# Regrouping the retention stage of a fused retention, MLP and gated-attention kernel into steps of whole head pairs

## The chip, the cores and the metric

One core of a Trainium2 chip runs the whole program. The metric is the device time of one execution in microseconds (us). The core has five engines that run side by side, each in its own order: TensorE (PE, matrix products; its weight loads are shown apart as PEld), VectorE (DVE), ScalarE (ACT), GpSimd (POOL), and SyncE (SP), which here only issues DMA transfers. Engines wait for each other on semaphores. Matrix products land in PSUM, eight banks of 512 fp32 columns in each of 128 partitions; DVE and ACT read PSUM, everything else lies in SBUF.

## The reference, cut to what matters

Three blocks follow one another. The change touches only the first, a retention (linear attention with decay) over 2 batches, 8 heads, 768 positions and 64 channels a head:

```python
gamma = 1.0 - 2.0 ** (-5.0 - np.arange(H))
for t in range(S):
    state = gamma * state + einsum('bhd,bhe->bhde', k[:, :, t], v[:, :, t])
    y[:, :, t] = scale * einsum('bhd,bhde->bhe', q[:, :, t], state)
x = y.transpose(0, 2, 1, 3).reshape(B, S, H * D)
# then: x + relu(layernorm(x) @ w_ch1) @ w_ch2, and a top-2 gated mixture of four causal attentions
```

All of it is fp32. The second block (layer norm, hidden layer of 2048, back to 512) starts when the retention's output is there.

## The kernel before

The retention is done in chunks of 128 positions (six a sequence). The decay is folded into the rows of q and k beforehand (`scale_rows`, L295: `scaled_k`, `scaled_q`), so inside a chunk the result is a causally masked score matrix times v, and over chunks it is q times a running sum of the chunks' k-v products. Two heads (a pair) lie side by side in the 128 partitions, so there are eight pairs (`NIT` = 8), and the six chunks of a pair are worked in two groups of three (`g` = 0, 1). For every pair `it`, TensorE does

- `turn(it, unit)`, L616: transposes of `scaled_k` and `scaled_q`, four units of three 128x128 tiles (units 0 and 1 belong to group 0, 2 and 3 to group 1). ACT copies each unit out of PSUM (`turned`, L956, into `k_t` and `q_t`).
- `scores_of(it, g)`, L629: three chunks x two heads, each a product over 64 rows (the array shape that the profile writes 64*128), the two heads side by side. DVE multiplies them by the causal mask (`apply_causal`, L1175, into `prob`).
- `chunk_outputs(it, g)`, L642: `prob` times v, each head into 64 of the 128 columns (shape 128*64), side by side.
- `key_values(it)`, L674: outer products k-v of five chunks x two heads, also 128*64. DVE makes the running sums from them (`states`, L1184 and L1187).
- `state_outputs(it, g)`, L649: q times the running sum, on the full array (128*128), added onto the chunk outputs in PSUM. ACT copies the sum out to `x` (`y_out`, L962).

An fp32 product appears in the profile as two matmul records and a transpose as one: 12 records for the scores or the chunk outputs of a group, 20 for `key_values`, 4 and 6 for the state outputs of groups 0 and 1, 3 for a transpose unit.

The order is written out by hand on every engine. Before the change the groups of two neighbouring pairs are interleaved: scores (it, 1), chunk outputs (it, 0), state outputs (it, 0), transposes of the next pair, scores (it+1, 0), chunk outputs (it, 1), key-values (it+1), state outputs (it, 1), transposes. Transposes use PSUM banks 0 and 1 in turn, all scores banks 2 and 3, outputs banks 4 and 5, key-values banks 6 and 7.

The rows of q, k and v come by DMA from SP (`load_heads`, L409), three pairs deep; `raw_v` of pair n is loaded once the state outputs of pair n-3 are finished (`s_y`). GpSimd scales the rows of pairs 2 to 7 (L295), then splits the weights of the MLP into high and low parts (L497 to L507); the splits of the second weight matrix start when all of `x` is out (`s_yx`). A first mean over channels (`first_mean`, L657), `first_centre` (L1244), `first_hi` (L974) and `first_lo` (L1250) prepare the MLP's first input tiles, and `hidden(0, 0)` (L723) is the MLP's first product. From there TensorE runs the MLP without a pause.

Of the kernel before, what the change touches and what calls it, by code (L numbers as in the profile page):

```python
# [70 lines left out]
def retention_moe_program(nc, q, k, v, g_ln, w_ch1, w_ch2, w_gate, wq, wk, wv, wo, out):  # L71
# [30 lines left out]
    with ExitStack() as ctx:  # L102
# [55 lines left out]
        with ExitStack() as r:  # L158
            raw = {n: sb(r, f"raw_{n}", [P, RB, 2, NC, D]) for n in "qkv"}
            scaled = {n: sb(r, f"scaled_{n}", [P, RB, NC, 2 * D]) for n in "qk"}  # L160
            k_t = sb(r, "k_t", [P, 2, NC, P])
            q_t = sb(r, "q_t", [P, 2, NC, P])
            prob = sb(r, "prob", [P, 2, 2, G, P])
            state = sb(r, "state", [P, 2, NC - 1, P])

        with ExitStack() as m:
            w2 = {part: sb(m, f"w2_{part}", [P, NF, DM], F32R) for part in ("hi", "lo")}
            h_t = {part: sb(m, f"h_t_{part}", [P, 2, N], F32R) for part in ("hi", "lo")}
            xn_t = {part: sb(m, f"xn_t_{part}", [P, KT, N], F32R) for part in ("hi", "lo")}
            rows = sb(m, "rows", [P, B, KT, U, P])  # L170
# [433 lines left out]
        def _(pe):  # L604

            def turn(n, unit):

                which, g = T_UNITS[unit]
                pe.wait_ge(s_scaled[which], 2 * n + g + 1)
                if unit >= 2:  # L610

                    pe.wait_ge(s_turned, 4 * n + unit - 1)
                elif n >= 1:
                    pe.wait_ge(s_turned, 4 * (n - 1) + unit + 3)
                for c in range(G):
                    mm = pe.transpose(t_bank(unit)[:, c * P:(c + 1) * P], scaled[which][:, n % RB, G * g + c, :],  # L616
                                      ident[:, :])
                mm.then_inc(s_t, 1)

            def scores_of(it, g):  # L620

                pe.wait_ge(s_turned, 4 * it + 2 * g + 2)
                if 2 * it + g >= 1:

                    pe.wait_ge(s_prob, 2 * it + g)
                for c in range(G):
                    for j in range(2):
                        rows = slice(j * D, (j + 1) * D)
                        mm = pe.matmul(s_bank()[:, j, c], k_t[rows, it % 2, G * g + c, :],  # L629
                                       q_t[rows, it % 2, G * g + c, :], start=True, stop=True)  # L630
                mm.then_inc(s_s, 1)

            def chunk_outputs(it, g):

                wait_loaded(pe, it, "v", g)
                pe.wait_ge(s_prob, 2 * it + g + 1)
                if it >= 1:
                    pe.wait_ge(s_yx, y_turn(it - 1, g) + 1)
                for c in range(G):
                    for j in range(2):  # L640
                        rows_ = slice(j * D, (j + 1) * D)
                        pe.matmul(y_bank(g)[rows_, c * P:(c + 1) * P], raw["v"][:, it % RB, j, G * g + c], prob[:, g, j, c, :],  # L642
                                  start=(c == 0), stop=(g == 0 and c == 0), skip_group_check=True)

            def state_outputs(it, g):

                pe.wait_ge(s_st, (NC - 1) * (it + 1))
                for c in range(max(1, G * g), G * g + G):
                    mm = pe.matmul(y_bank(g)[:, (c - G * g) * P:(c - G * g + 1) * P], state[:, it % 2, c - 1, :],  # L649
# [3 lines left out]
            def first_mean(b):  # L653

                pe.wait_ge(s_const, 5)
                pe.wait_ge(s_acc, (HP - 1) * (b + 1))
# [29 lines left out]
            for it in range(NIT - 1):  # L686

                scores_of(it, 1)
                chunk_outputs(it, 0)
                if it == NIT - 2:  # L690
                    key_values(it + 1)
                state_outputs(it, 0)
                if it == HP + 1:
                    first_mean(0)
                for unit in range(0 if it == 0 else 2, 4):
                    turn(it + 1, unit)

                scores_of(it + 1, 0)
                chunk_outputs(it, 1)
                if it < NIT - 2:  # L700
                    key_values(it + 1)
                    state_outputs(it, 1)
                    for unit in (0, 1):
                        turn(it + 2, unit)

            chunk_outputs(NIT - 1, 0)
            state_outputs(NIT - 1, 0)
            state_outputs(NIT - 2, 1)
            scores_of(NIT - 1, 1)
            first_mean(1)  # L710
            chunk_outputs(NIT - 1, 1)
            state_outputs(NIT - 1, 1)
# [45 lines left out]
            hidden(0, 0)  # L758
            hidden(0, 1)
            pe.wait_ge(s_yx, 2 * NIT)  # L760
# [186 lines left out]
        def _(act):  # L947
# [11 lines left out]
            def y_out(it, g):  # L959

                act.wait_ge(s_y, y_turn(it, g) + 1)
                act.activation(x[:, it, G * g:G * g + G, :].rearrange("p c t -> p (c t)"), y_bank(g),  # L962
# [21 lines left out]
            for it in range(NIT - 2):  # L984
                y_out(it, 0)
                for unit in range(0 if it == 0 else 2, 4):
                    turned(it + 1, unit)
                y_out(it, 1)
                for unit in (0, 1):
                    turned(it + 2, unit)  # L990
                if it == HP + 1:
                    for kk in range(KT):
                        first_hi(0, kk)
            y_out(NIT - 2, 0)
            for unit in (2, 3):
                turned(NIT - 1, unit)
            y_out(NIT - 1, 0)
            y_out(NIT - 2, 1)
            for kk in range(KT):
                first_hi(1, kk)  # L1000
            y_out(NIT - 1, 1)
# [166 lines left out]
        def _(dve):  # L1168

            def apply_causal(it, g):  # L1170
                dve.wait_ge(s_s, 2 * it + g + 1)
                if it >= 1:

                    dve.wait_ge(s_y, y_turn(it - 1, g) + 1)
                dve.tensor_tensor(prob[:, g], s_bank(),  # L1175
# [22 lines left out]
            states(0)  # L1198

# [144 lines left out]
            for it in range(NIT - 1):  # L1344
                apply_causal(it, 1)
                if it == 0:
                    dve.wait_ge(s_tab_rest, 16)
                    for g in range(2):
                        for n in "kq":
                            scale_rows(dve, 1, n, g)  # L1350
                if it == NIT - 2:
                    states(it + 1)
                b, kk = divmod(it - 1, HP)
                if it >= 2 and kk > 0:
                    first_sum(b, kk)
                if it == HP + 1:
                    for kk in range(KT):
                        first_centre(0, kk)
                apply_causal(it + 1, 0)
                if it < NIT - 2:  # L1360
                    states(it + 1)
            first_sum(1, HP - 2)
            for kk in range(KT):
                first_lo(0, kk)
            first_sum(1, HP - 1)
            apply_causal(NIT - 1, 1)
# [192 lines left out]
```

## Time and profile before

| | |
|---|---|
| median of 3 runs | 471.7 us (471.1 to 472.78) |
| the profiled execution | 470.56 us, of which the span is 468.8 us |
| PE busy | 456.1 us (97%) |
| DVE, ACT, POOL busy | 269.7, 149.9, 153.2 us |
| retention: first transpose to first MLP product | 5.1 to 64.3 us of the span |
| granted TensorE clock | 1.00 throughout |

The span goes from the first to the last instruction; the rest of the time of the execution lies around it. A busy PE is one that always has a matmul in flight. A matmul's record lasts longer than it blocks the next, so a group's duration in the timeline overlaps the following group; the chain of waits, in which each piece ends where the next begins, shows what a group really takes.

### The profile page before, as it was taken

Reading aid. Unit: us, or ns where it says so; the run is one execution under the profiler, and the core shown is the slowest. Engines: PE = TensorE matmul, PEld = TensorE weight load, DVE = VectorE, ACT = ScalarE, POOL = GpSimd, SP = SyncE. Lnnn points to the kernel's source line nnn. Section 1 sums busy time; section 2 is a strip of 40 time slices with the busy share of each in tenths; the row PEclk is TensorE's granted clock in tenths of the full one; section 3 lists DMA queues with packets and bytes.
Section 4 is the critical chain, followed back from the end, with each engine's and each line's share of the span. In section 5 each row is a group of like instructions: output and inputs, shape, how many; then the busy total and the mean of one; then the engine's idle time right before and its main releaser. Section 6 shows DMA issues by size and latency. Waiting matters only on the chain.

```text
span 468.8 us, 7454 instructions
## 1 busy us (share of the span) xinstructions
PE 456.1 (97%) x2762; PEld 392.8 (84%) x2762; DVE 269.7 (58%) x599; ACT 149.9 (32%) x343; POOL 153.2 (33%) x190
## 2 busy tenths in 40 slices
PE   7999999999999999999999999999999899999896
PEld 6788878888888888888888888888999799998775
DVE  4555761186515388732265785144438889888833
ACT  2434431111113111111131111132435777777823
POOL 1474438998900000000002000000501667666710
PEclk9999999999999999999999999999999999999999
DMA  7997504344200000000040000000155444442024
GB/s 170 245 216 161 142 23 136 112 136 134 67 1 1 0 0 0 0 0 0 0 101 13 0 1 0 0 2 0 24 127 123 119 117 107 99 103 68 1 111 159
DMA packets 65792, 33.04 MB, mean 70 GB/s; under 512 B 47584, under 2 KB 61920, under 8 KB 65760
## 3 DMA queue, kind: packets, MB, share of 16 engines
q1 hardware_dynamic: 64960, 32.43, 26.8%
q8 instruction: 19, 0.31, 0.3%
q10 hardware_dynamic: 800, 0.20, 0.2%
q14 instruction: 13, 0.11, 0.1%
HBM read 20.03 MB, written 3.15 MB: 49 GB/s over the span
## 4 chain that ended last, share of the span: by engine, by line
PE 87%; DVE 5%; ACT 2%; issue 2%; SPq 1%; DMA 1%; POOL 1%; POOLq 0%; ACTq 0%; DVEq 0%
PE ps L723 28%; PE ps L732 28%; PE ps L807 5%; PE ps L858 4%; PE ps L779 3%; PE ps L826 3%; PE ps L642 3%; PE ps L629 3%; PE ps L841 2%; PE ps L649 2%; PE ps L885 2%; PE ps L616 2%; DVE a L1439 2%; SPq L445 1%; DVE a_low_lo L1447 1%
## 5 line engine op out<-in xcount | busy, mean ns | idle before, releaser
L1290 DVE SCALAR_TENSOR_TENSOR h_t_lo<-ps,h_t_hi 128x512 fp32r<-128x512 f32 x48 | 33.2, 692 | 124.5 <-ACT h_t_hi L1011 124.5
L1011 ACT ACTIVATE h_t_hi<-ps 128x512 fp32r<-128x512 f32 x48 | 28.7, 598 | 216.7 <-PE ps L723 216.7
L723 PE MATMUL ps<-xn_t_hi,w_hi 128*128 128x512 f32 x192 | 74.9, 390 | 0.0
L723 PE MATMUL ps<-xn_t_lo,w_hi 128*128 128x512 f32 x192 | 74.8, 390 | 0.0
L732 PE MATMUL ps<-w_hi,h_t_lo 128*128 128x512 f32 x192 | 74.8, 390 | 0.0
L723 PE MATMUL ps<-xn_t_hi,w_lo 128*128 128x512 f32 x192 | 74.8, 390 | 0.0
L732 PE MATMUL ps<-w_hi,h_t_hi 128*128 128x512 f32 x192 | 74.8, 390 | 0.0
L732 PE MATMUL ps<-w_lo,h_t_hi 128*128 128x512 f32 x192 | 74.8, 390 | 0.0
L574 POOL TENSOR_SCALAR a<-a,inv_den,weight 128x768 f32<-128x768 f32 (+5 forms) x48 | 34.0, 717 | 50.6 <-DVE inv_den L1459 50.3
L723 PEld LDWEIGHTS ps<-xn_t_hi,w_hi 128*128 128x128 f32 x192 | 36.1, 188 | 7.6
L723 PEld LDWEIGHTS ps<-xn_t_hi,w_lo 128*128 128x128 f32 x192 | 36.1, 188 | 7.5
L732 PEld LDWEIGHTS ps<-w_hi,h_t_lo 128*128 128x128 f32 x192 | 36.1, 188 | 7.5
L732 PEld LDWEIGHTS ps<-w_hi,h_t_hi 128*128 128x128 f32 x192 | 36.1, 188 | 7.5
L732 PEld LDWEIGHTS ps<-w_lo,h_t_hi 128*128 128x128 f32 x192 | 36.1, 188 | 7.4
L723 PEld LDWEIGHTS ps<-xn_t_lo,w_hi 128*128 128x128 f32 x192 | 36.1, 188 | 7.3
L537 POOL TENSOR_SCALAR w_vg_hi<-raw_vg 128x1040 fp32r<-128x1040 f32 x1 | 1.1, 1061 | 118.5 <-DMA raw_wo<-in_moe_wo 118.5
L1066 ACT ACTIVATE a<-a,neg_max 128x768 f32<-128x768 f32 (+5 forms) x48 | 32.3, 674 | 13.9 <-DVE neg_max L1439 13.9
L1277 DVE STREAM_TRANSPOSE rows<-x 32x512 f32<-32x512 f32 x48 | 33.7, 702 | 1.4
L1439 DVE CUSTOM_DVE_ANT_0 a<-ps,masked 128x768 f32<-128x768 f32 (+5 forms) x48 | 27.8, 616 | 0.3 <-PE ps L826 0.3
L841 PE MATMUL ps<-ident,a 128*128 128x128 f32 x168 | 23.6, 277 | 3.5 <-DVE a_low_lo L1447 2.4
L545 POOL TENSOR_SCALAR raw_qk<-raw_qk 128x256 f32<-128x256 f32 x4 | 1.6, 405 | 77.4 <-PE ps L732 76.7
L841 PEld LDWEIGHTS ps<-ident,a 128*128 128x128 f32 x168 | 18.6, 141 | 6.6 <-POOL a L574 5.0
(146 smaller groups left out, 891.2 us busy)
## 6 DMA issues: line engine op xcount, KB each, us to landing
raw_w<-in_moe_w_ch SPq DMA_DIRECT2D x32, 256.0 KB, 2.9
k_twice_hi<-pj_hi SPq DMA_DIRECT2D x32, 96.0 KB, 2.2
k_twice_lo<-pj_lo SPq DMA_DIRECT2D x32, 96.0 KB, 2.2
out_y<-out_sb SPq DMA_DIRECT2D x12, 256.0 KB, 2.0
raw_k<-in_k SPq DMA_DIRECT2D x7, 384.0 KB, 4.7
raw_q<-in_q SPq DMA_DIRECT2D x7, 384.0 KB, 5.2
raw_v<-in_v SPq DMA_DIRECT2D x7, 384.0 KB, 3.8
q_both<-pj_hi SPq DMA_DIRECT2D x16, 96.0 KB, 2.1
```

What stands on the lines that cost most here:

```text
L574: pool.tensor_scalar(a[:, g % AB, c0:c1], a[:, g % AB, c0:c1], inv_den[:, u:u + 1], weight[:, u, e:e + 1], ALU.mult, ALU.mult).then_inc(s_ ...
L629: mm = pe.matmul(s_bank()[:, j, c], k_t[rows, it % 2, G * g + c, :], q_t[rows, it % 2, G * g + c, :], start=True, stop=True)
L723: mm = pe.matmul(ps[:, f % 2, :], w1[a_][:, f, kk, :], xn_t[b_][:, kk, :], start=(kk == 0 and p_ == 0), stop=(kk == KT - 1 and p_ == 2))
L732: mm = pe.matmul(ps[:, 2 + tau, :], h_t[a_][:, f % 2, tau * P:(tau + 1) * P], w2[b_][:, f, :], start=(f == 0 and p_ == 0), stop=(f == NF - ...
L807: mm = pe.matmul(pj_bank(n), w_qk[a_][n // 4 % 2][:, kk, :], x2[b_][:, b, kk, half_cols(n)], start=(kk == 0 and p_ == 0), stop=(kk == KT - ...
L841: mm = pe.transpose(flat(4, 6, s0 + P)[:, s0:s0 + P], a[:, g % AB, s0:s0 + P], ident[:, :])
L858: mm = pe.matmul(z_bank(top)[:, skip:HALF], ev[:, b * NC + sc, e].rearrange("p h d -> p (h d)"), (a_top if top else a_low)[part][:, sc, sk ...
L1011: act.activation(h_t["hi"][:, f % 2, :], ps[:, f % 2, :], ACT.Relu).then_inc(s_hhi, 1)
L1066: act.activation(a[:, g % AB, c0:c1], a[:, g % AB, c0:c1], ACT.Exp, bias=neg_max[:, 2 * (g % AB) + w:2 * (g % AB) + w + 1], scale=-1.0, ac ...
L1277: dve.transpose(rows[quad(a_), :, :, :, quad(d_)].rearrange("p b k u d -> p (b k) u d"), x[quad(d_), :, U * n:U * n + U, quad(a_)]).then_i ...
L1290: dve.scalar_tensor_tensor(h_t["lo"][:, f % 2, :], ps[:, f % 2, :], 0.0, f32(h_t["hi"][:, f % 2, :]), ALU.max, ALU.subtract).then_inc(s_hl ...
L1439: dve.tensor_tensor_reduce(a[:, g % AB, c0:c1], sc_bank(g, c1)[:, c0:c1], masked[:, NC - 1 - i:NC, :].rearrange("p c t -> p (c t)"), -1.0, ...
```

## The change

The retention runs in steps of a whole pair. A step's order on TensorE is: scores of both groups of pair `it`, chunk outputs of both groups of the pair before, key-values of `it`, state outputs of both groups of the pair before, the four transpose units of pair `it+1`. Pair 0 is finished before step 1 begins, and pairs 6 and 7 are finished together at the end. Transpose units take banks 0 to 3, one each, and the scores of group g banks 2g and 2g+1; so a transpose now waits for the masking (`s_prob`) that reads the scores in its banks, and `prob` is kept for two pairs. ACT and DVE follow: ACT copies out both output groups and then the four units, DVE masks both groups and then makes the running sums. The outputs of pair 7 go to banks 0 and 1, so the wait for all of `x` moves ahead of `hidden(0, 1)`. `rows` and `xn_t` change places in SBUF.

```diff
-            prob = sb(r, "prob", [P, 2, 2, G, P])
+            prob = sb(r, "prob", [P, 2, 2, 2, G, P])
...
         def t_bank(unit):
-            return ps[:, unit % 2, 0:G * P]
+            return ps[:, unit, 0:G * P]
-        def s_bank():
-            return ps[:, 2:4, 0:G * P].rearrange("p j (c t) -> p j c t", c=G)
+        def s_bank(g):
+            return ps[:, 2 * g:2 * g + 2, 0:G * P].rearrange("p j (c t) -> p j c t", c=G)
-        def y_bank(g):
-            return ps[:, 4 + g, 0:G * P]
+        def y_bank(it, g):
+            return ps[:, (0 if it == NIT - 1 else 4) + g, 0:G * P]
...
                 pe.wait_ge(s_scaled[which], 2 * n + g + 1)
-                if unit >= 2:
-                    pe.wait_ge(s_turned, 4 * n + unit - 1)
-                elif n >= 1:
-                    pe.wait_ge(s_turned, 4 * (n - 1) + unit + 3)
+                if n >= 1:
+                    pe.wait_ge(s_prob, 2 * n - 1 + unit // 2)
...
                 pe.wait_ge(s_turned, 4 * it + 2 * g + 2)
-                if 2 * it + g >= 1:
-                    pe.wait_ge(s_prob, 2 * it + g)
...
             key_values(0)
-            for it in range(NIT - 1):
-                scores_of(it, 1)
-                chunk_outputs(it, 0)
-                if it == NIT - 2:
-                    key_values(it + 1)
-                state_outputs(it, 0)
+            scores_of(0, 1)
+            for g in range(2):
+                chunk_outputs(0, g)
+                state_outputs(0, g)
+            for unit in range(4):
+                turn(1, unit)
+            for it in range(1, NIT - 1):
+                for g in range(2):
+                    scores_of(it, g)
+                if it > 1:
+                    for g in range(2):
+                        chunk_outputs(it - 1, g)
+                key_values(it)
+                if it > 1:
+                    for g in range(2):
+                        state_outputs(it - 1, g)
+                for unit in range(4):
+                    turn(it + 1, unit)
                 if it == HP + 1:
                     first_mean(0)
-                for unit in range(0 if it == 0 else 2, 4):
-                    turn(it + 1, unit)
-                scores_of(it + 1, 0)
+            for g in range(2):
+                scores_of(NIT - 1, g)
+            key_values(NIT - 1)
+            for it in (NIT - 2, NIT - 1):
+                chunk_outputs(it, 0)
+            for it in (NIT - 2, NIT - 1):
+                state_outputs(it, 0)
+            for it in (NIT - 2, NIT - 1):
                 chunk_outputs(it, 1)
...
             first_mean(1)
-            chunk_outputs(NIT - 1, 1)
-            state_outputs(NIT - 1, 1)
+            for it in (NIT - 2, NIT - 1):
+                state_outputs(it, 1)
...
             hidden(0, 0)
+            pe.wait_ge(s_yx, 2 * NIT)
             hidden(0, 1)
-            pe.wait_ge(s_yx, 2 * NIT)
...
-            for it in range(NIT - 2):
-                y_out(it, 0)
-                for unit in range(0 if it == 0 else 2, 4):
-                    turned(it + 1, unit)
-                y_out(it, 1)
-                for unit in (0, 1):
-                    turned(it + 2, unit)
+            for it in range(1, NIT):
...
+                if it != 2:
+                    for g in range(2):
+                        y_out(max(0, it - 2), g)
+                for unit in range(4):
+                    turned(it, unit)
...
-            for it in range(NIT - 1):
-                apply_causal(it, 1)
...
-                apply_causal(it + 1, 0)
-                if it < NIT - 2:
-                    states(it + 1)
+            for it in range(1, NIT):
...
+                apply_causal(it, 0)
+                if it < NIT - 1:
+                    apply_causal(it, 1)
+                states(it)
...
+            apply_causal(NIT - 1, 1)
             first_sum(1, HP - 2)
-            for kk in range(KT):
-                first_lo(0, kk)
             first_sum(1, HP - 1)
-            apply_causal(NIT - 1, 1)
```

On TensorE, the order of one whole period in the middle of the retention before (one group of pair `it`, then the other; the name says what is read, `q_t,k_t` are scores, `prob,raw_v` chunk outputs, `raw_v,scaled_k` key-values, `q_t,state` state outputs, `ident,...` transposes):

```order
L629 MATMUL ps<-q_t,k_t 128x128 x6
L642 MATMUL ps<-prob,raw_v 64x128 x6
L649 MATMUL ps<-q_t,state 128x128 x2
L616 MATMUL ps<-ident,scaled_k 128x128 x3
L616 MATMUL ps<-ident,scaled_q 128x128 x3
L629 MATMUL ps<-q_t,k_t 128x128 x6
L642 MATMUL ps<-prob,raw_v 64x128 x6
L674 MATMUL ps<-raw_v,scaled_k 64x64 x10
L649 MATMUL ps<-q_t,state 128x128 x3
L616 MATMUL ps<-ident,scaled_k 128x128 x3
L616 MATMUL ps<-ident,scaled_q 128x128 x3
```

and the same place after:

```order
L623 MATMUL ps<-q_t,k_t 128x128 x12
L636 MATMUL ps<-prob,raw_v 64x128 x12
L670 MATMUL ps<-raw_v,scaled_k 64x64 x10
L643 MATMUL ps<-q_t,state 128x128 x5
L613 MATMUL ps<-ident,scaled_k 128x128 x3
L613 MATMUL ps<-ident,scaled_q 128x128 x3
L613 MATMUL ps<-ident,scaled_k 128x128 x3
L613 MATMUL ps<-ident,scaled_q 128x128 x3
```

The same instructions stand there, but scores, chunk outputs and state outputs come once in a period instead of twice, and all transposes of a pair stand directly ahead of its scores.

On ACT in the same place, before (`k_t` and `q_t` are the transposes' copies, `x` an output group's):

```order
L962 ACTIVATE x<-ps 128x384
L956 ACTIVATE k_t<-ps 128x384
L956 ACTIVATE q_t<-ps 128x384
L962 ACTIVATE x<-ps 128x384
L956 ACTIVATE k_t<-ps 128x384
L956 ACTIVATE q_t<-ps 128x384
```

and after:

```order
L965 ACTIVATE x<-ps 128x384 x2
L959 ACTIVATE k_t<-ps 128x384
L959 ACTIVATE q_t<-ps 128x384
L959 ACTIVATE k_t<-ps 128x384
L959 ACTIVATE q_t<-ps 128x384
```

Six copies stand in a row now, the outputs' ahead of the four of the transposes.

## Rows read from the trace of the kernel before

**Rows 1.** The page, busy time, share of the span and instructions of each engine
```profile
PE 456.1 (97%) x2762; PEld 392.8 (84%) x2762; DVE 269.7 (58%) x599; ACT 149.9 (32%) x343; POOL 153.2 (33%) x190
```
**Rows 2.** Chain of waits, 24 to 31 us: start, us until the next piece, what
```profile
24.22 0.87 PE ps L649 x6
25.08 0.65 PE ps L616 x6
25.74 0.87 PE ps L629 x12
26.61 0.81 PE ps L642 x12
27.41 0.64 PE ps L649 x4
...
30.38 0.58 PE ps L674 x20
```
**Rows 3.** Windows, one period: us, busy PE PEld DVE ACT POOL, clock, DMA
```profile
24.90:31.70 6.80, 6.80 (x93) 5.99 (x92) 3.74 (x9) 2.51 (x6) 4.51 (x6) 1.00 1.01 231
```
**Rows 4.** Timeline of PE: start, us, line, out<-in, array shape, count
```profile
24.15 0.94 PE L649 MATMUL ps<-q_t,state 128*128 128x128 f32 x6
...
26.54 0.88 PE L642 MATMUL ps<-prob,raw_v 128*64 128x128 f32 x12
...
27.34 0.71 PE L649 MATMUL ps<-q_t,state 128*128 128x128 f32 x4
...
29.51 0.88 PE L642 MATMUL ps<-prob,raw_v 128*64 128x128 f32 x12
...
30.21 0.75 PE L674 MATMUL ps<-raw_v,scaled_k 128*64 128x64 f32 x20
```
**Rows 5.** Timeline of ACT's copies out of PSUM, and one handoff to PE
```profile
6.12 0.49 ACT L956 ACTIVATE q_t<-ps 128x384 f32<-128x384 f32 x1
...
6.66 0.94 PE L629 MATMUL ps<-q_t,k_t 64*128 64x128 f32 x12 [0.58 <-ACT q_t L956]
...
25.12 0.49 ACT L962 ACTIVATE x<-ps 128x384 f32<-128x384 f32 x1 [2.52 <-PE ps L649]
...
25.51 0.48 ACT L956 ACTIVATE k_t<-ps 128x384 f32<-128x384 f32 x1
...
25.88 0.50 ACT L956 ACTIVATE q_t<-ps 128x384 f32<-128x384 f32 x1
```
**Rows 6.** Timeline of DVE, running sums and masking
```profile
24.59 1.27 DVE L1187 TENSOR_TENSOR state<-ps,state 128x128 f32<-128x128 f32 x4
...
26.65 0.96 DVE L1175 TENSOR_TENSOR prob<-ps,causal 128x768 f32<-128x768 f32 x1 [0.80 <-PE ps L629]
```
**Rows 7.** Timeline of the start, 11 to 20 us
```profile
11.36 0.95 DVE L1175 TENSOR_TENSOR prob<-ps,causal 128x768 f32<-128x768 f32 x1
...
13.76 0.55 DVE L295 TENSOR_TENSOR scaled_q<-raw_q,decay_sb 128x384 f32<-128x384 f32 x1
...
19.14 0.83 POOL L295 TENSOR_TENSOR scaled_q<-raw_q,decay_sb 128x384 f32<-128x384 f32 x1
```
**Rows 8.** Timeline of SP and POOL, one load and the scaling behind it
```profile
38.61 0.37 SPq L409 DMA_DIRECT2D raw_v<-in_v  x1
...
47.71 0.83 POOL L295 TENSOR_TENSOR scaled_q<-raw_q,decay_sb 128x384 f32<-128x384 f32 x1
```
**Rows 9.** Timeline of the end of the retention
```profile
61.67 0.70 PE L657 MATMUL ps<-head_sum,mean_of 128*128 128x256 f32 x2
...
62.66 0.74 DVE L1244 TENSOR_TENSOR centred<-x,ps 128x256 f32<-128x256 f32 x2
...
62.84 0.88 PE L642 MATMUL ps<-prob,raw_v 128*64 128x128 f32 x12 [0.48 <-issue]
...
64.34 0.47 PE L723 MATMUL ps<-xn_t_hi,w_hi 128*128 128x512 f32 x1
...
66.20 0.62 POOL L505 TENSOR_SCALAR w_hi<-raw_w 128x512 fp32r<-128x512 f32 x1 [12.09 <-ACT x L962]
```

More of the change, by code:

```diff
@@ L168, in retention_moe_program @@
             h_t = {part: sb(m, f"h_t_{part}", [P, 2, N], F32R) for part in ("hi", "lo")}
+            rows = sb(m, "rows", [P, B, KT, U, P])
             xn_t = {part: sb(m, f"xn_t_{part}", [P, KT, N], F32R) for part in ("hi", "lo")}
-            rows = sb(m, "rows", [P, B, KT, U, P])
             stats = sb(m, "stats", [P, NT, 2, 6])
@@ L628, in scores_of @@
                         rows = slice(j * D, (j + 1) * D)
-                        mm = pe.matmul(s_bank()[:, j, c], k_t[rows, it % 2, G * g + c, :],
+                        mm = pe.matmul(s_bank(g)[:, j, c], k_t[rows, it % 2, G * g + c, :],
                                        q_t[rows, it % 2, G * g + c, :], start=True, stop=True)
@@ L648, in state_outputs @@
                 for c in range(max(1, G * g), G * g + G):
[L649 removed]
+                    mm = pe.matmul(y_bank(it, g)[:, (c - G * g) * P:(c - G * g + 1) * P], state[:, it % 2, c - 1, :],
                                    q_t[:, it % 2, c, :], start=False, stop=True, skip_group_check=True)
@@ L983, in _ @@
                 turned(0, unit)
-            for it in range(NIT - 2):
-                y_out(it, 0)
-                for unit in range(0 if it == 0 else 2, 4):
-                    turned(it + 1, unit)
-                y_out(it, 1)
-                for unit in (0, 1):
-                    turned(it + 2, unit)
-                if it == HP + 1:
+            for it in range(1, NIT):
+                if it == HP + 3:
                     for kk in range(KT):
                         first_hi(0, kk)
[L994 to L998, printed above, removed]
+                if it != 2:
[3 more added lines that the diff above has]
+                    turned(it, unit)
+            for it in (NIT - 2, NIT - 1):
+                y_out(it, 0)
             for kk in range(KT):
                 first_hi(1, kk)
-            y_out(NIT - 1, 1)
+            for it in (NIT - 2, NIT - 1):
+                y_out(it, 1)
             def xn_hi(n, kk):
@@ L1198, in _ @@
             states(0)
+            apply_causal(0, 1)
+            dve.wait_ge(s_tab_rest, 16)
+            for g in range(2):
+                for n in "kq":
+                    scale_rows(dve, 1, n, g)
             def normalise(n):
@@ L1342, in mlp @@
                     hidden_lo(i + 1, 1)
-            for it in range(NIT - 1):
-                apply_causal(it, 1)
[L1346 to L1351, printed above, removed]
-                    states(it + 1)
-                b, kk = divmod(it - 1, HP)
+            for it in range(1, NIT):
+                if it == HP + 2:
+                    for kk in range(KT):
+                        first_centre(0, kk)
+                if it == HP + 3:
+                    for kk in (2, 3):
+                        first_lo(0, kk)
+                b, kk = divmod(it - 2, HP)
                 if it >= 2 and kk > 0:
                     first_sum(b, kk)
-                if it == HP + 1:
-                    for kk in range(KT):
-                        first_centre(0, kk)
-                apply_causal(it + 1, 0)
-                if it < NIT - 2:
-                    states(it + 1)
+                apply_causal(it, 0)
+                if it < NIT - 1:
+                    apply_causal(it, 1)
+                states(it)
+                if it == HP + 2:
+                    for kk in (0, 1):
+                        first_lo(0, kk)
+            apply_causal(NIT - 1, 1)
             first_sum(1, HP - 2)
-            for kk in range(KT):
-                first_lo(0, kk)
             first_sum(1, HP - 1)
-            apply_causal(NIT - 1, 1)
             first_centre(1, 0)
```

21 lines of the change are left out of this document (8 added, 13 removed).

## The prediction, made before the changed kernel was run

> **What bounds the kernel now.** I read the page's busy shares first, then the chain of waits through the retention, then PE's timeline in it. The page has PE busy for 97% of the span [rows 1], so only what shortens PE's own work or its pauses can shorten the kernel. The chain of waits runs through nothing but PE in the middle of the retention, and in one period there (two groups of a pair) PE is busy for the whole stretch, ACT for 2.5 us of 6.8 [rows 3]. The reader should see in [rows 2] that pieces of like work cost unlike times. State outputs take 0.64 us for four records and 0.87 for six, so a record costs 0.11 and 0.20 to 0.21 is left over. Six transposes take 0.65, which is 6 x 0.11 with nothing over. Twelve score records, two side by side, are six slots of 0.11 and take 0.87: 0.21 over. Chunk outputs are also six slots and take 0.81: 0.15 over. The key-values take 0.58 for ten slots of half width, nothing over. What the three with something over share is that each begins with another array shape than the work ahead of it had: full array to 64*128, to 128*64, back to the full array. The two without follow work of their own shape. [Rows 4] shows it with the same work twice: chunk outputs go on to key-values, of their own shape, after 0.70 us (29.51 to 30.21), but to state outputs, of another, after 0.80 (26.54 to 27.34); the rest of the extra sits behind the first record of the new shape. So a change of shape costs about 0.10 as a pause and 0.05 to 0.10 in the first product.
>
> The sum of a period: 2 x 0.87 + 2 x 0.81 + 0.58 + 0.64 + 0.87 + 2 x 0.65 = 6.75, of which 2 x (0.21 + 0.15 + 0.20) = 1.1 us is changes of shape.
>
> The Trainium skill, page "TensorEngine Tiling (Array Packing)", section Tiling Modes, says that a change of the tiling mode, unlike a change of tile, drains the engine. By that rule grouping by shape saves whatever the drains cost, and the rows above give the price; the same page's section Performance Considerations speaks against the change, see the first rival.
>
> **The steady step.** The change keeps every instruction and halves the changes of shape: 6.75 - 0.55 = 6.2 us a step if PE still never waits. Laid out from the first score at 0: scores to 1.44, pause, chunk outputs 1.54 to 2.91, key-values to 3.49, pause, state outputs 3.59 to 4.81, transposes to 6.12, next scores at 6.22.
>
> Does anything make PE wait?
> - Masking (DVE): group 0's scores are done at about 0.93, group 1's at 1.61; each masking takes 0.96 [rows 6], so both are done by 2.9. The transposes that now wait for it, and behind which everything on PE would queue, come at 4.81. Hidden.
> - Running sums (DVE): key-values are done at 3.66, the sums take 0.3 + 1.27 [rows 6] and end at 5.3; the state outputs that need them come in the next step at 3.6. Hidden.
> - Copies (ACT): this is the tight one. Before, the transposes of a group stood about 3 us ahead of the scores that use them; now the scores of group 0 come directly behind. The last state output is done at 4.97 (a record is in flight for 0.28: 24.15 + 0.94 less the start of the last record, 5 x 0.11 + 0.1 behind the first) [rows 4]. Both output copies stand ahead of the transposes' on ACT. ACT starts a copy 0.03 after the product is done (24.15 + 0.94 against 25.12) [rows 4, 5] and a next one 0.39 and 0.37 after the last, although each is shown as 0.48 to 0.50 [rows 5]. So: second output copy at 5.01, first k copy at 5.40, first q copy at 5.77, done at 6.26, and PE starts 0.05 later as at 6.12 + 0.49 = 6.61 against 6.66 [rows 5]: 6.31. The scores start at 6.31 instead of 6.22: 0.1 us a step is given back. Group 1's copies are done at 7.0, its scores are due at 7.08: hidden.
>
> So a step takes 6.3 us. The upper bound of this unknown: if six copies in a row went one after the other at 0.49, group 0's would be done at 6.48 and group 1's at 7.46; the scores of group 0 would start at 6.53, those of group 1 at 7.5 instead of 7.3, and a step would cost 6.75. The lower bound is 6.2. I take 6.3, since a pitch of 0.37 to 0.39 is what three copies in a row show, the third of which was ready to go before ACT was.
>
> **Start.** Nothing changes up to the masking of pair 0's second group. The second chunk outputs of pair 0 wait for the masking of 11.36 + 0.95 = 12.31 [rows 7]: 12.36 to 13.07; state outputs 13.17 to 13.94. The transposes of pair 1 follow at 13.94; their rows are all scaled by 13.76 + 0.55 = 14.31, the last unit's 0.6 us ahead of its turn, so PE no longer waits unit by unit. They end at 15.25; the copies behind the two output copies free the scores at 15.44. Scores to 16.89, key-values to 17.6. The transposes of pair 2 then wait for GpSimd's scaling, which is bound by its loads and does not move: its last unit is scaled at 19.14 + 0.83 = 19.97 [rows 7], so they end at 20.35 and step 2 starts at 20.44. Bounds: 20.3 and 20.9 (a load or the copies later).
>
> **Steps 2 to 6.** 20.44 + 6.31 = 26.75, then 33.06 and 39.37. Step 5 has the first mean (two records of 256 columns, 0.44 at 0.11 for 128) behind the transposes, which also gives ACT time to catch up: 39.37 + 6.22 + 0.43 = 46.02. Its centring (four operations on DVE, two of which take 0.74 [rows 9], so 1.4) makes the maskings of step 6 0.8 us later, against 2.4 us of slack. Step 7 starts at 52.33.
>
> **End.** Steps of the last order, from 52.33: scores to 1.44, key-values 1.54 to 2.17, chunk outputs of group 0 of both pairs to 3.49, state outputs 3.59 to 4.59 (the sums of pair 7 are done at 4.0, hidden), chunk outputs of group 1 4.69 to 6.05 (masking done at 4.9, hidden, where the kernel before waits at 62.84 [rows 9]), mean 6.15 to 6.69, state outputs to 8.03. The centring can start 0.05 behind the mean's 0.70 in flight [rows 9], at 6.90; before, the MLP's first product came 64.34 - 62.66 = 1.68 behind the first centring [rows 9], with PE as the last to be ready; without that I count 1.55: 8.45. PE waits 0.4 us there for the first input tile. The first product is at 52.33 + 8.45 = 60.8 instead of 64.34: 3.5 us earlier.
>
> **Behind it.** The wait for all of `x` ahead of `hidden(0, 1)`: the split that waits for it started 66.20 - 62.66 = 3.54 behind the first centring [rows 9]; with one more copy (0.39) it is 3.93, less 1.55 is 2.4 us behind the first product, whose group of twelve needs 2.7: hidden by 0.3. GpSimd's split itself takes 0.62 and a second part of about twice that, to 4.3; it is needed at 5.5: hidden. The loads' order on SP is unchanged; `raw_v` of pair n is released a step later by its order, but steps are shorter. From the MLP on PE is the bound as before, so the 3.5 us reach the end. The swap in SBUF costs nothing, since no transfer or operand changes in size. In the profiled execution: span 468.8 - 3.5 = 465.3, time 470.56 - 3.5 = 467.1. That execution lies 1.1 us under the median of the runs, so from the median 471.7 - 3.5 = **468.2 us**.
>
> **Rivals.**
> - *The copies pace the step* (15%). The upper bound above: 0.45 us more in each of steps 2 to 4 and 6, and 0.3 at the start and the end: 2.1 us given back, 470.3 us or a little less. For it: a copy is shown as 0.49, and six in a row are nowhere in the trace. Against it: the pitch of three. Even so it is not slower than before. The page "TensorEngine Tiling (Array Packing)" of the Trainium skill, section Performance Considerations, warns that tiling speeds up the products but not the copies out of PSUM, which may become the bound; here the trace has ACT busy for 2.5 of 6.8 us [rows 3], so by load they do not; the bound above is one of latency, at one place.
> - *The extra belongs to the start of a group, not to the shape* (7%). Each group also starts with a wait on a semaphore. Then a step stays at 6.75 and only the start and the end gain: 471.3 us. Against it: the transposes behind state outputs and the key-values behind chunk outputs start with such waits too and have nothing over.
> - *The loads fall behind* (5%), the one on the slower side. A pair's v load now waits for outputs that finish one step later in the order, and k and q of the next pair queue behind it on SP, GpSimd's scaling behind them, and the transposes behind that. Before, the scaling for pair 7 ends 47.71 + 0.83 - 38.61 = 9.9 us after that v load was issued [rows 8]. After, the v load goes out 5.0 into a step and the last transposes that need the scaling are due 5.8 into the step two later: 2 x 6.3 + 0.8 = 13.4 us. It decides once that chain takes over 13.4; with 15.5 us for each of the pairs 5 to 7 it costs over 6 us and ends at 474 us. Against it: 3.5 us of slack.
> - *Less is lost than I count* (8%): the steps run at 6.2 and the end's wait of 0.4 is filled: 0.4 + 0.4 more, 467.4 us.
>
> **Numbers.** My forecast, with small errors of either sign, has 65%; its own range is 467.2 to 469.3. With the first rival inside, the range is 466.8 to 470.8. About 0.3% (1.4 us) is what a measurement of this kernel can tell from none. Faster by more (under 470.3): the forecast, the last rival and two thirds of the first: 0.84. Within: 0.11. Slower: 0.05.
>
> **What would show it.** In PE's timeline: one group of 24 score records, 24 of chunk outputs, 20, 10 and 12 in a row, at a distance of 6.2 to 6.4 us from step to step, the pieces 1.5, 1.4, 0.6, 1.2 and 1.3. A pause named after ACT's `q_t` of about 0.1 (wrong if 0.3 or more) ahead of the scores, the first score of step 2 near 20.4, the first MLP product near 60.8. Steps of 6.7 without waits would refute the price of the shapes; waits for `scaled_k` or `scaled_q` behind step 2 would show the loads.

## The result, and the profile after

The changed kernel is slower by 0.5%: 474.38 us (median of 8 runs, 472.57 to 476.1) against 472.19 us of the kernel before beside it (8 runs, 471.1 to 473.26), a ratio of 1.0047 [1.0026, 1.0069]. The prediction was 468.2 us, faster. The profiled execution took 474.35 us with a span of 472.6.

The page's line of busy time, which answers to [rows 1], gives PE half a microsecond less work in a span 3.8 us longer. So PE waits more, or the marks at both ends moved:

```profile
PE 455.6 (96%) x2762; PEld 394.4 (83%) x2762; DVE 268.8 (57%) x599; ACT 149.6 (32%) x343; POOL 153.6 (32%) x190
```

I then read the chain of waits of the changed kernel. Its middle, which answers to [rows 2]:

```profile
27.62 1.71 PE ps L623 x24
29.33 1.46 PE ps L636 x24
30.79 0.58 PE ps L670 x20
31.37 1.31 PE ps L643 x10
32.68 1.31 PE ps L613 x12
...
34.02 1.71 PE ps L623 x24
...
48.28 5.25 DMA g_col<-in_moe_g_ln
...
53.96 1.29 ACT xn_t_hi L977 x3
55.26 0.75 ACT x L965 x2
56.00 0.38 ACT k_t L959
56.38 0.39 ACT q_t L959
...
56.81 2.41 PE ps L623 x24
59.22 1.26 PE ps L670 x20
```

The reader is to see two things. In the middle a step is 6.40 us (27.62 to 34.02), against 6.75 before, and its pieces are close to the ones that were forecast. At 45.5 us the chain leaves PE, which it never did there before. It goes through SP's issues to the load of `g_col`, the gain of the layer norm (512 numbers), from there to `first_hi` on ACT, the two output copies, two transposes' copies, and only then to PE's scores of pair 7. Those 24 score records take 2.41 us instead of 1.71, and the 20 key-values 1.26 instead of 0.58.

One step by windows of the changed kernel, which answers to [rows 3] (us, busy PE, PEld, DVE, ACT, POOL, clock, DMA). ACT is as busy as before, 2.51 us, now in 6.40:

```profile
27.60:34.00 6.40, 6.37 (x90) 5.92 (x90) 3.86 (x8) 2.51 (x7) 4.75 (x6) 1.00 0.81 185
```

The timeline of the changed kernel, which answers to [rows 4 to 9]: the start and the end of step 2, the wait, and the first MLP product:

```profile
19.95 0.83 POOL L295 TENSOR_TENSOR scaled_q<-raw_q,decay_sb 128x384 f32<-128x384 f32 x1
...
21.32 1.61 PE L623 MATMUL ps<-q_t,k_t 64*128 64x128 f32 x24
...
26.31 0.49 ACT L965 ACTIVATE x<-ps 128x384 f32<-128x384 f32 x1 [0.18 <-PE ps L643]
26.70 0.49 ACT L959 ACTIVATE k_t<-ps 128x384 f32<-128x384 f32 x1
27.07 0.50 ACT L959 ACTIVATE q_t<-ps 128x384 f32<-128x384 f32 x1
27.44 0.51 ACT L959 ACTIVATE k_t<-ps 128x384 f32<-128x384 f32 x1
27.62 1.71 PE L623 MATMUL ps<-q_t,k_t 64*128 64x128 f32 x24
27.81 0.53 ACT L959 ACTIVATE q_t<-ps 128x384 f32<-128x384 f32 x1
...
47.02 0.53 ACT L959 ACTIVATE q_t<-ps 128x384 f32<-128x384 f32 x1
...
53.55 1.71 ACT L977 ACTIVATE xn_t_hi<-centred,g_col 128x256 fp32r<-128x256 f32 x4 [6.00 <-DMA g_col<-in_moe_g_ln]
...
56.81 2.41 PE L623 MATMUL ps<-q_t,k_t 64*128 64x128 f32 x24 [3.38 <-ACT q_t L959]
...
66.96 0.47 PE L726 MATMUL ps<-xn_t_hi,w_hi 128*128 128x512 f32 x1 [0.33 <-DVE xn_t_lo L1255]
```

ACT is done with pair 6's transposes at 47.5, reaches `first_hi` and stands there for 6.00 us until `g_col` is in. Behind it in ACT's order are the output copies of pair 5 and all transposes' copies of pair 7, so PE stands for 3.38 us. In the kernel before, `first_hi` stood behind the output copies of pair 5 and the first two transposes' copies of pair 7. The same load was issued at about the same time there (48.13 against 48.28) and landed after 4.2 us, at 52.3; ACT came to `first_hi` at 53.66 and found it there (timeline of before, no time in brackets ahead of the last row):

```profile
48.13 0.43 SPq L452 DMA_DIRECT2D g_col<-in_moe_g_ln  x1
...
53.66 1.71 ACT L974 ACTIVATE xn_t_hi<-centred,g_col 128x256 fp32r<-128x256 f32 x4
```

Windows of 2 us of the changed kernel, PE alone (us, busy PE, granted clock, DMA share, GB/s):

```profile
54.00:56.00 2.00, 0.00 (x0) 1.00 0.45 130
56.00:58.00 2.00, 1.19 (x16) 0.90 0.00 0
58.00:60.00 2.00, 2.00 (x28) 0.50 0.00 0
60.00:62.00 2.00, 2.00 (x34) 0.75 0.00 0
```

After the pause the granted clock stays full for the first records, falls to 0.50 (1.2 of 2.4 GHz) for somewhat over 3 us and comes back at 61. That is why the score and key-value records of step 7 take longer. The Trainium skill, page "TensorE: Matmul & The Clock Gate", section What's actually happening, says that TensorE is throttled to half its clock unless it has lately been active; the trace agrees, the fall comes behind a pause of 3.38 us (`e2` below has one behind shorter waits).

The first MLP product comes at 66.96 instead of 64.34 [rows 9], 2.6 us later, and every later piece of PE is shifted by the same 2.6. The other 1.2 us by which the two spans differ lie behind the last work of DVE (468.24 + 0.69 us against 465.60 + 0.69), in the last output transfer, which the order doesn't touch.

### The profile page after: what moved, and what is told of

It is laid out like the page before. It is cut to its first block, busy times and chain, and to the rows that moved or that the text cites. A ratio compares the mean times of both kernels' runs of the same rounds, so it can differ in the third digit from the quotient of the medians.

```text
span 472.6 us, 7436 instructions
## 1 busy us (share of the span) xinstructions
PE 455.6 (96%) x2762; PEld 394.4 (83%) x2762; DVE 268.8 (57%) x599; ACT 149.6 (32%) x343; POOL 153.6 (32%) x190
## 4 chain that ended last, share of the span: by engine, by line
PE 82%; DVE 5%; SPq 3%; DMA 3%; ACT 3%; issue 2%; POOL 1%; POOLq 0%; ACTq 0%; DVEq 0%
PE ps L726 28%; PE ps L735 28%; PE ps L810 5%; PE ps L861 4%; PE ps L782 3%; PE ps L829 3%; PE ps L844 2%; PE ps L888 2%; PE ps L623 2%; PE ps L636 2%; DVE a L1441 2%; PE ps L643 1%; DMA raw_q<-in_q 1%; DMA g_col<-in_moe_g_ln 1%; SPq L445 1%
## 5 line engine op out<-in xcount | busy, mean ns | idle before, releaser
L1066 ACT ACTIVATE a<-a,neg_max 128x768 f32<-128x768 f32 (+5 forms) x48 | 32.3, 674 | 13.9 <-DVE neg_max L1441 13.9
```

What stands on the lines that cost most here:

```text
L1066: act.activation(a[:, g % AB, c0:c1], a[:, g % AB, c0:c1], ACT.Exp, bias=neg_max[:, 2 * (g % AB) + w:2 * (g % AB) + w + 1], scale=-1.0, ac ...
```

## The experiments

Each has a short name, in brackets in its heading. The ratio of each is to the kernel before on the same chip (471.59 us, 35 runs, and 471.68, 29 runs, for `e4`, `e6`, `e8` and `e9`). The marks "..." in the diffs stand for lines left out. Times inside a kernel are from its profile; two marks serve throughout, the first score of step 7 and the first MLP product, 56.81 and 66.96 in the changed kernel.

**The load of `g_col` earlier, in the changed kernel (`e1`).** The load goes behind those of pair 5.

```diff
                 load_heads(it)
+                if it == 5:
...
+                        sp.dma_start(g_col[:, :], g_ln.rearrange("(k p) -> p k", p=P)).then_inc(s_gcol, 16)
...
-                sp.dma_start(g_col[:, :], g_ln.rearrange("(k p) -> p k", p=P)).then_inc(s_gcol, 16)
```

> The changed kernel with one edit: the 2 KB load of the gains g_col is issued behind the loads of pair 5 instead of behind the loads of the weights. Theory (the wait for g_col): in the changed kernel ACT's first_hi(0, 0) stands ahead of the output copies of pair 5 and the four transposes' copies of pair 7, and waited for g_col until 53.5 us; PE then had nothing to do for 3.4 us and came back at the lower clock. Expected: no wait for g_col, no pause ahead of step 7, granted clock 1.00 throughout, first MLP product at about 47.2 + 6.4 + 8.5 = 62.1 us instead of 66.96, so 4.9 us less than the changed kernel: about 469.5 us, 0.6% under the kernel before. Rival (the new order itself starves PE, the load is only what came last): the pause stays or moves, 473 to 474.5 us.

Measured: 469.82 us, ratio 0.9964 [0.9951, 0.9978]. One small transfer turns 0.5% slower into 0.4% faster. Step 7 starts at 53.36, 3.45 us earlier, and the first MLP product stands at 62.80, 4.16 earlier; the clock is full throughout. From the timeline of this kernel:

```profile
47.67 1.71 ACT L978 ACTIVATE xn_t_hi<-centred,g_col 128x256 fp32r<-128x256 f32 x4 [0.24 <-DVE centred L1250]
...
52.26 3.32 DVE L1256 SCALAR_TENSOR_TENSOR xn_t_lo<-centred,g_col,xn_t_hi 128x256 fp32r<-128x256 f32 x4
...
56.92 0.88 PE L637 MATMUL ps<-prob,raw_v 128*64 128x128 f32 x12 [0.47 <-DVE prob L1176]
...
62.80 0.47 PE L727 MATMUL ps<-xn_t_hi,w_hi 128*128 128x512 f32 x1 [0.33 <-DVE xn_t_lo L1256]
```

`first_hi` waits 0.24 us instead of 6.00. But the end, from 53.36, takes 9.44 us, not the 8.45 forecast: the four `first_lo` on DVE take 3.32 us, and behind them the masking of pair 7 is late, for which PE waits 0.47. This is the subject of `e8`.

**The load as it is, its users later, in the changed kernel (`e2`).** ACT's and DVE's work on the first batch's input tiles goes behind the loop over the pairs.

```diff
             for it in range(1, NIT):
-                if it == HP + 3:
-                    for kk in range(KT):
-                        first_hi(0, kk)
...
+            for kk in range(KT):
+                first_hi(0, kk)
             for it in (NIT - 2, NIT - 1):
                 y_out(it, 0)
...
-                        first_lo(0, kk)
...
             first_sum(1, HP - 1)
+            for kk in range(KT):
+                first_lo(0, kk)
```

> The changed kernel with g_col loaded where it was, but its users moved: first_hi(0, .) on ACT behind all transposes' copies, first_lo(0, .) on DVE behind the last first_sum. Theory (the wait for g_col): g_col still lands at about 53.5 us, but nothing that PE needs stands behind it on ACT, so step 7 starts at about 53.6 with the clock at 1.00; the four first_lo at the end make the last centring 0.4 to 0.5 us later: first MLP product at about 62.5, 469.9 us. Rival (the new order starves PE by itself): 473 to 474.5 us.

Measured: 470.13 us, ratio 0.9968 [0.9954, 0.9982]. Step 6 takes 6.31 us (49.14 to 55.45) instead of 9.65, at full clock. The load isn't harmful in itself; what stands behind its user in ACT's order is. The first MLP product is at 64.47, 1.67 later than in `e1`, and the reason lies at the start, as the timeline and a window of this kernel show:

```profile
21.89 2.94 PE L623 MATMUL ps<-q_t,k_t 64*128 64x128 f32 x24
...
22.00:24.00 2.00, 2.00 (x20) 0.50 1.15 262
```

The second step begins 0.68 us later than in `e1` (21.89 against 21.21) and takes 7.71 us instead of 6.30, since the granted clock is 0.50 for some 3.4 us of it. Ahead of it PE had waited three times for GpSimd's scaled rows, 1.00, 0.24 and 0.24 us; `e9` has waits of 0.54, 0.75, 0.24 and 0.24 us there and keeps its clock at 1.00. The end is 0.42 shorter than in `e1` (9.02 against 9.44), although PE waits 0.76 for the last input tiles. This execution (471.65 us) and one of 471.8 us have a mean granted clock of 0.995, the other ten of 0.997 or more, and they took 470.92 us or less. So most of them are without that fall.

**The same earlier load in the kernel before (`e3`).** The diff is that of `e1`.

> The kernel before with g_col issued behind the loads of pair 5. Theory (the wait for g_col): there g_col had landed at 52.3 us and its first user came at 53.66, so the wait was covered by 1.3 us and taking it earlier is worth nothing: the same 472.2 us within 0.3%. Rival (the small load disturbs the large ones around it, wherever it is put): a difference of 0.5 us or more either way, and loads of pair 6 that land later.

Measured: 471.57 us, ratio 1.0002 [0.999, 1.0014]. So an earlier `g_col` is worth nothing in the old order, and all that it gives in `e1` belongs to the new one.

**The load later in the kernel before (`e4`).** Its issue waits until the running sums of pair 6 are there.

```diff
+            sp.wait_ge(s_st, (NC - 1) * (HP + 3))
                 sp.dma_start(g_col[:, :], ...)
```

> The kernel before with g_col issued only when the running sums of pair 6 are done (about 53.3 us) instead of at 48.1. Theory (an early user on ACT exposes a late load, in either order): it lands at about 56, first_hi(0, 0) waits from 53.7 to 56, the output copy and the transposes' copies behind it on ACT come some 2 us later than at 56.1, and PE waits for them: 1.5 to 3 us slower than the kernel before, 473 to 474.6. Rival (the order before has so much slack behind first_hi that a late load costs nothing, the new order alone is to blame): within 0.3% of the kernel before.

Measured: 471.1 us, ratio 0.9997 [0.998, 1.0015]. The timeline of this kernel:

```profile
53.12 0.37 SPq L453 DMA_DIRECT2D g_col<-in_moe_g_ln  x1
...
55.23 1.71 ACT L975 ACTIVATE xn_t_hi<-centred,g_col 128x256 fp32r<-128x256 f32 x4 [1.63 <-DMA g_col<-in_moe_g_ln]
56.85 0.47 ACT L963 ACTIVATE x<-ps 128x384 f32<-128x384 f32 x1
```

ACT does wait for `g_col`, 1.63 us, and it costs nothing: the output copy behind it starts at 56.85 instead of 56.09, and the first MLP product is at 64.16. I had held that the load is exposed in either order once it is late; that fell as far as this run goes. In the old order ACT has idle time behind `first_hi`, and PE wants the transposes' copies late: the last of them is done at 58.07, and the scores that read it start at 60.61. The delay came out shorter than meant, since the lone load landed in 2.1 us; a longer one was not tried.

**The pause filled, in the changed kernel (`e5`).** PE makes 30 transposes into a free part of a bank while it waits. The wait for `g_col` stays.

```diff
                     first_mean(0)
+            pe.wait_ge(s_st, (NC - 1) * (NIT - 1))
+            pe.wait_ge(s_xc, KT)
+            for _ in range(30):
+                pe.transpose(ps[:, 7, 3 * P:4 * P], ident[:, :], ident[:, :])
             for g in range(2):
                 scores_of(NIT - 1, g)
```

> The changed kernel with 30 transposes of the identity into a free part of bank 7 ahead of step 7, where PE has nothing to do while ACT waits for g_col. Theory (two costs, a pause of 3.4 us and then a lower clock worth 1.7 us in the last steps): the pause stays, the clock stays at 1.00, the last steps take 8.5 us instead of 10.15: 1.7 us less than the changed kernel, about 472.7 us. Rival (the last steps are slow because ACT and DVE are late, not because of the clock): unchanged at 474.4 us, or slower by what the transposes get in the way.

Measured: 473.03 us, ratio 1.004 [1.0027, 1.0053]. Two rows of the timeline and one window of this kernel, all engines:

```profile
53.95 1.71 ACT L981 ACTIVATE xn_t_hi<-centred,g_col 128x256 fp32r<-128x256 f32 x4 [5.92 <-DMA g_col<-in_moe_g_ln]
...
352.29 0.47 PE L833 MATMUL ps<-k_twice_hi,q_both 128*128 128x512 f32 x1 [1.27 <-issue]
...
58.00:60.00 2.00, 2.00 (x46) 1.88 (x44) 1.25 (x2) 0.00 (x0) 0.00 (x0) 1.00 0.04 8
```

The clock stays full, and the end (57.22 to 65.81) takes 8.59 us against 10.15: the halved clock cost 1.56. Step 7 begins 0.41 later than in the changed kernel, and that isn't the filler's doing: `g_col` came later (its issue at 48.98 instead of 48.28), `first_hi` starts 0.40 later, and the last filler ends at 57.19, the copy that the scores wait for at 57.16. The first MLP product is 1.15 us earlier. In the profiled execution that is lost again far behind, where PE stands for 1.27 us ahead of an attention product and the changed kernel doesn't; the profile names no releaser, and the spans are 472.4 and 472.6 us. The ratios, 1.0047 [1.0026, 1.0069] and 1.004 [1.0027, 1.0053], don't separate the two kernels either. So the price of the lower clock rests on this stretch of the two profiles; step 2 of `e2` has about the same, 1.41 us for some 3.4 us at 0.50.

**The changes of shape put back, on top of `e1` (`e6`).** Scores of a group and chunk outputs of a group alternate again.

```diff
                 for g in range(2):
                     scores_of(it, g)
-                if it > 1:
-                    for g in range(2):
+                    if it > 1:
                         chunk_outputs(it - 1, g)
```

> The changed kernel with g_col early (as e1), and in steps 1 to 6 the order scores group 0, chunk outputs group 0, scores group 1, chunk outputs group 1: two more changes of array shape in each of steps 2 to 6, the same instructions and the same number of waits. Theory (each change of shape costs 0.15 to 0.2 us): steps of 6.6 to 6.75 us instead of 6.4, some 1.2 to 1.7 us more than e1, about 471.3 us. Rival (the extra belongs to the start of a group, whatever its shape): as e1, 469.8 us.

Measured: 471.31 us, ratio 0.9986 [0.9974, 0.9998], 0.2% behind `e1`. The same work on PE in other order (timeline of this kernel):

```profile
34.94 0.94 PE L624 MATMUL ps<-q_t,k_t 64*128 64x128 f32 x12
35.81 0.88 PE L637 MATMUL ps<-prob,raw_v 128*64 128x128 f32 x12
36.61 0.94 PE L624 MATMUL ps<-q_t,k_t 64*128 64x128 f32 x12
37.48 0.88 PE L637 MATMUL ps<-prob,raw_v 128*64 128x128 f32 x12
38.19 0.75 PE L671 MATMUL ps<-raw_v,scaled_k 128*64 128x64 f32 x20
...
41.59 0.60 PE L624 MATMUL ps<-q_t,k_t 64*128 64x128 f32 x6
```

and in the timeline of `e1`:

```profile
33.92 1.71 PE L624 MATMUL ps<-q_t,k_t 64*128 64x128 f32 x24
...
36.91 0.75 PE L671 MATMUL ps<-raw_v,scaled_k 128*64 128x64 f32 x20
```

A step is 6.65 us (34.94 to 41.59) instead of 6.40. The difference is all in scores and chunk outputs: 3.25 us up to the key-values at 38.19, against 2.99 (33.92 to 36.91). Of the 2.99, 0.1 is a wait for the second group's copies, which the interleaved order hides. So two more changes of shape cost 0.25 a step net and 0.35 by themselves; at 0.21 and 0.15 the prediction priced them at 0.36.

**`first_lo` away from GpSimd's splits, on top of `e1` (`e8`).** The first one goes behind the first masking of pair 7, the other three behind the last sum but one.

```diff
                 apply_causal(it, 0)
                 if it < NIT - 1:
                     apply_causal(it, 1)
+                else:
+                    first_lo(0, 0)
...
-                        first_lo(0, kk)
...
+            for kk in range(1, KT):
+                first_lo(0, kk)
```

> The changed kernel with g_col early (as e1), and the four first_lo of the first half moved on DVE: one behind the masking of pair 7's first group, three behind the last first_sum. In e1 they took 0.90 us each instead of 0.48 where GpSimd was splitting weights beside them, and held the masking of pair 7 up. Theory (DVE and GpSimd slow each other there, and DVE is late): 0.48 us each at the new places, no wait of the chunk outputs of pair 7, the last order takes 8.5 to 8.7 us instead of 9.4: about 469.0 us. Rival (first_lo is slow for what it reads, wherever it stands): 0.9 us each at the new places too, the end 9.4 us or more, 469.8 or worse.

Measured: 469.5 us, ratio 0.9958 [0.9945, 0.9971]. On DVE and PE in the timeline of this kernel:

```profile
55.26 0.47 DVE L1256 SCALAR_TENSOR_TENSOR xn_t_lo<-centred,g_col,xn_t_hi 128x256 fp32r<-128x256 f32 x1
...
59.22 1.27 DVE L1256 SCALAR_TENSOR_TENSOR xn_t_lo<-centred,g_col,xn_t_hi 128x256 fp32r<-128x256 f32 x3
...
62.03 0.47 PE L727 MATMUL ps<-xn_t_hi,w_hi 128*128 128x512 f32 x1 [0.36 <-DVE xn_t_lo L1256]
```

One `first_lo` takes 0.47, three take 1.27, PE no longer waits for the masking, and the end takes 8.63 us (53.40 to 62.03) instead of 9.44. In time it and `e1` can't be told apart; the mark moved by 0.8 us.

**Transposes further ahead of their scores, on top of `e8` (`e9`).** The transposes of the next pair go ahead of the state outputs, the copies of `q_t` are kept three deep for it, and ACT copies the transposes first (its new order is left out of the diff).

```diff
-            q_t = sb(r, "q_t", [P, 2, NC, P])
+            q_t = sb(r, "q_t", [P, 3, NC, P])
...
                 key_values(it)
+                for unit in range(4):
+                    turn(it + 1, unit)
                 if it > 1:
                     for g in range(2):
                         state_outputs(it - 1, g)
-                for unit in range(4):
-                    turn(it + 1, unit)
...
-                if n >= 2:
-                    act.wait_ge(s_y, y_turn(n - 2, g) + 1)
+                if n >= 3 and which == "q":
+                    act.wait_ge(s_y, y_turn(n - 3, g) + 1)
+                if n >= 2 and which == "k":
+                    act.wait_ge(s_s, 2 * (n - 2) + g + 1)
```

> As e8, and in every step the four transpose units stand ahead of the state outputs (of the same array shape), with ACT's copies in that order and q_t kept for three pairs instead of two. Theory (the 0.1 to 0.2 us a step that PE waits at the scores are the copies' latency): no wait ahead of either group's scores, steps of 6.2 us instead of 6.4 in steps 3 to 6, 0.8 us less than e8: about 468.2 us. Rival (steps are held by something else, such as the scaled rows): steps stay at 6.3 to 6.4, as e8.

Measured: 469.14 us (6 runs, 468.58 to 469.55), ratio 0.994 [0.9924, 0.9955], the fastest version and 0.6% under the kernel before. PE in the middle, and one place of the end, from the timeline of this kernel:

```profile
28.06 1.61 PE L624 MATMUL ps<-q_t,k_t 64*128 64x128 f32 x24
...
34.22 1.61 PE L624 MATMUL ps<-q_t,k_t 64*128 64x128 f32 x24
...
54.49 1.28 POOL L500 TENSOR_TENSOR w_lo<-raw_w,w_hi 128x512 fp32r<-128x512 f32 x1
54.98 1.07 DVE L1261 SCALAR_TENSOR_TENSOR xn_t_lo<-centred,g_col,xn_t_hi 128x256 fp32r<-128x256 f32 x1
```

A step is 6.16 us without a wait of PE, and the scores take 1.61. Its first MLP product is at 62.07, no earlier than in `e8`, since its second step began late (21.90) and the end took 8.95 with one `first_lo` beside a split again. Its lead over `e8` lies inside the intervals.

## Why the prediction was wrong

The direction was wrong, and the step that failed is the sentence on the centring in step 5, with step 6 put at 6.31 us behind it. The change moves `first_centre` on DVE and `first_hi` on ACT ahead of copies that PE waits for, and the prediction asked only for DVE's slack (2.4 us). It never asked what the moved instruction on ACT waits for, nor what is queued behind it; that wait stands in the sum at nothing. It wrote "The loads' order on SP is unchanged" and took that as harmless, but it was the ACT side that moved towards a load that stayed. The runs show a step longer by 3.34 us in its place, all of it a wait, and 1.56 us of lower clock behind it. Point by point, the first MLP product at 66.96 instead of 60.8:

- *Price of the shapes: right.* Steps are 6.40 instead of 6.75 us; without waits (`e9`) they are 6.16, and 6.2 was the forecast for that; putting two changes back costs 0.25 to 0.35 (`e6`), forecast 0.36. The rival that the extra belongs to the start of a group is refuted.
- *Copies on ACT: right in kind, 0.09 short a step.* The pitch of 0.37 to 0.39 holds for the five that stand in a row in the step (26.31, 26.70, 27.07, 27.44, 27.81) and for all six behind the wait for `g_col` (55.16 to 57.01), and the first wait ahead of the scores comes as forecast: step 2 takes 6.30 (21.32 to 27.62). In steps 3 and 4, "Group 1's copies are done at 7.0, its scores are due at 7.08: hidden" is what missed. The fourth copy is shown as 0.53 and done at 28.34, and what waits for it is a weight load, which goes ahead of the product that the prediction looked at: the first one of group 1's scores starts at 28.39, where the pace of 0.11 of the ones before would have it at 28.28. The score records take 1.71 instead of 1.61. With a step 5 of 6.73 instead of 6.65 this makes 0.26 us.
- *Start: 0.88 late.* GpSimd's last scaling for pair 2 starts at 19.95 instead of 19.14 [rows 7]. The first score of step 2 is at 21.32, outside the bounds given (20.3 to 20.9). The load of pair 2 that it waits for last is issued at about the same time (12.1 to 12.6 us in all profiles) and takes 5.6 to 6.3 us to land in the profiles with the new order against 4.9 to 5.2 in the three with the old. What delays it isn't settled: no run aimed at it. A 16 KB transfer on the instruction queue stands beside these loads, between 13.9 and 16.2 us in the new order and between 16.3 and 17.0 in the old; whether it has to do with it was not tried.
- *Step 6: 9.65 instead of 6.31.* The wait for `g_col`; 3.34 us. `e1` and `e2` remove it from two sides, each to 6.31, `e3` shows that the old order has no such wait to lose, and `e4` that a wait of 1.63 us at this place costs it nothing.
- *End: 10.15 instead of 8.45.* Of the 1.70, 1.56 are the halved clock behind the pause (`e5`), a consequence of the same wait. The sum of the end was right otherwise: 8.59 in `e5`, 8.63 in `e8`.

Together 0.88 + 0.26 + 3.34 + 1.70 = 6.2 us, all of the miss in the profile. The rival on the slower side had the right end (474 us) by luck, with another mechanism; the loads of the pairs never held PE up behind the start of step 2. The rival that the copies pace the step at 6.75 didn't occur.

With the wait gone the change gives 0.4% (`e1`), 1.8 us of the 3.5 that were forecast. In its profile the first MLP product is 1.54 us earlier than before instead of 3.5; the rest went to the start (0.8), the steps (0.3) and the end (1.0, of which `e8` has 0.8 back by moving `first_lo` away from the splits).

## What to carry to other kernels

When an order is rewritten, list for every engine each instruction that now comes earlier relative to its neighbours, with what it waits for and what is queued behind it, loads included: here a transfer of 2 KB stopped an engine that was 32% busy and through it the one that was 96% busy. A parameter load behind bulk loads is cheap to issue early. Count a pause of PE with what the clock may cost behind it, here half as much again.

## What the runs showed of the hardware that was not expected

- A pause of 3.4 us on PE was followed by a little over 3 us at half clock, which cost 1.56 us; with 30 filler transposes in the pause the clock stayed at 1.00 (`e5`).
- Shorter waits can do the same: in `e2` the granted clock fell to 0.50 for some 3.4 us behind waits of 1.00, 0.24 and 0.24 us, and that step took 7.71 us instead of 6.30. Behind waits of 0.54, 0.75, 0.24 and 0.24 us at the same place (`e9`) it stayed at 1.00.
- The load of `g_col`, 2 KB in rows of 4 bytes, took 5.25 us (4.2 in the kernel before) from its issue to landing behind the weight loads, and 2.1 us when nothing had been issued for some time before it (`e4`).
- `first_lo`, two tensors read from SBUF, takes 0.47 us by itself (`e8`) and 1.07 beside GpSimd's split (`e9`), and four of them take 3.32 in `e1`. Masking, which reads PSUM and one tensor of SBUF, stayed at 0.96 beside the split. The Trainium skill, page "SBUF — State Buffer", section Who interferes with whom, says that a DVE instruction with two SBUF inputs takes the second through a read interface shared with GpSimd and so contends with a GpSimd instruction that reads SBUF, and that one with at most one SBUF input, outside certain fast modes, doesn't; the trace agrees for both instructions. If `first_lo` had stood still for the whole of the split in `e9`, it would have ended at 54.49 + 1.28 + 0.48 = 56.25, an estimate from these rows; it was done at 56.05.
